# Writing out TensorE's six-turn loop in a three-stage fused kernel

## The chip, the cores and the metric

The kernel runs on one core of a Trainium2 chip. The metric is the device time of one execution in microseconds; lower is better. Five engines of the core work side by side, each with its own instruction stream: TensorE (PE; its weight loads are PEld), VectorE (DVE), ScalarE (ACT), GpSimd (POOL) and SyncE (SP). They meet only through semaphores.

## The reference

```
x = attn(x, weight)                     # 7-tap causal mix over the sequence, softmaxed taps, per head
h1 = x @ moe_w_in                       # 192 -> 2048
g1 = h1 if h1 >= 1, 0 if h1 <= -1, else (h1 + 1)**2 / 4
y  = g1 @ moe_w_out                     # 2048 -> 192
h2 = y @ moe2_w_in                      # 192 -> 2048
g2 = s * relu(h2)**2 + b
out = g2 @ moe2_w_out                   # 2048 -> 192
```

There are 2 sequences of 4096 tokens with 192 channels, all in float32.

## The kernel before

The tokens are cut into 8 blocks of 512 per sequence (`NB = 8`, `T = 512`), both sequences side by side. Channels lie on the partitions. A *phase* is one layer (0 or 1) over one block. It runs over 16 chunks of 128 hidden units. For precision each float32 operand is split into a high part and a low part, and each product is made of several matmuls with 64-row operands. Two of them, on the two halves of the array, run at the same time: below, such a couple is called a *pair*.

In a phase TensorE walks the chunks two at a time. Here this is called a *group*: `up_pair` makes the hidden values of chunks j and j+1 (`up_own` twice, 5 pairs each, L670; `up_other` twice, 4 pairs each, L683) into the two PSUM tensors `h`, and `down` twice (10 pairs each, L717 and L732) multiplies chunks j-2 and j-1 by the second weight matrix into `acc` and `acc_rem`. So a group is 38 pairs, a phase is 8 groups, and the last two chunks of a phase are finished in the first group of the next one. Between the two, ACT makes `r` from `h` (L289 for layer 0, L291 for layer 1), DVE makes `g` (L445, L453; L447 for layer 1), ACT rounds it to `g_hi` (L303, L305) and DVE makes the rest `g_lo` (L463, L466). DVE also does the 7-tap mix of a later block (L498, L502), ACT and DVE split layer 0's result into layer 1's operands, and both drain the accumulators in the first group of a phase (L312 to L316 and L475, L478).

The order is written by hand. Phase (0, block 0) and phase (0, block 1) come first as straight code. Then a loop runs `LOOPS = NB - 2 = 6` times; each turn is one phase of layer 1 and one of layer 0 for a later block. The last two phases, both of layer 1, are straight code again. PE, DVE and ACT each have this loop, as a hardware loop (`Fori`) over a register; SP has one of five turns for its loads and stores. The loops of the engines are not tied to each other by anything but the semaphores of the data. All semaphore counts rise through the whole kernel, and a wait in a loop compares with a value worked out from the loop's register, where one in straight code compares with a constant.

Of the kernel before, what the change touches and what calls it, by code (L numbers as in the profile page):

```python
# [32 lines left out]
def build(nc, x, weight, w1_in, w1_out, w2_in, w2_out, s, b, out):  # L33
# [10 lines left out]
    LOOPS = NB - 2  # L44
# [3 lines left out]
    with ctx:  # L48
# [607 lines left out]
        def _(pe):  # L656
# [85 lines left out]
            def phase(layer, before, S0, P0, xs, split, weights=None):  # L742

                for j in range(0, CH, 2):
                    if weights and j in weights:
                        pe.wait_ge(w1_lo_done, weights[j])
                    up_pair(layer, j, S0 + j, xs, split if j == 0 else None)
                    for d in (j - LAG, j - LAG + 1):
                        if d >= 0:
                            down(layer, d, S0 + d, P0)  # L750
                        elif before is not None:
                            down(before, CH + d, S0 + d, P0 - 1)

            def mixed_split(blk):

                return {"hi": [(x_hi_done[0], blk + 1)], "lo": [(x_lo_done[0], blk + 1)],
                        "rem": [(x_rem_lo_done[0], 2 * (blk + 1))]}

            def y_split(blk):

                return {"hi": [(x_hi_done[1], blk + 1)], "lo": [(x_lo_done[1], blk + 1)],
                        "rem": [(x_rem_lo_done[1], 2 * (blk + 1))]}
# [23 lines left out]
            phase(0, None, 0, 0, X1, first_split, weights)  # L786
            phase(0, 0, CH, 1, X1, mixed_split(1))
            pe.wait_ge(w2_lo_done, N_PARTS)
            with pe.Fori(0, LOOPS) as c:
                S0, P0 = (c + 1) * (2 * CH), (c + 1) * 2  # L790
                phase(1, 0, S0, P0, X2, y_split(c))
                phase(0, 1, S0 + CH, P0 + 1, X1, mixed_split(c + 2))
# [31 lines left out]
```

## Time and profile before

| | us |
|---|---|
| median of 3 runs | 1169.5 (1169.03 to 1171.97) |
| the profiled execution's own time | 1166.02 |
| its span, from the first to the last instruction | 1164.3 |
| mean granted TensorE clock, as a share of full | 0.992 |
| busy: PE / PEld / DVE / ACT | 1126.6 / 983.3 / 947.4 / 630.3 |

The profiled execution took 1.7 us more than its span and 3.5 us less than the median of the runs. Busy time of PE counts the pipelined, modelled length of matmuls, so it shows where PE has work and not how well it is used. Idle time is listed by what ended it; "issue" is idle time for whose end the profile shows no other engine's event.

### The profile page before, as it was taken

Reading aid. Unit: us, or ns where it says so; the run is one execution under the profiler, and the core shown is the slowest. Engines: PE = TensorE matmul, PEld = TensorE weight load, DVE = VectorE, ACT = ScalarE, POOL = GpSimd, SP = SyncE. Lnnn points to the kernel's source line nnn. Section 1 sums busy time; section 2 is a strip of 40 time slices with the busy share of each in tenths; the row PEclk is TensorE's granted clock in tenths of the full one; section 3 lists DMA queues with packets and bytes.
Section 4 is the critical chain, followed back from the end, with each engine's and each line's share of the span. In section 5 each row is a group of like instructions: output and inputs, shape, how many; then the busy total and the mean of one; then the engine's idle time right before and its main releaser. Section 6 shows DMA issues by size and latency. Waiting matters only on the chain.

```text
span 1164.3 us, 23819 instructions
## 1 busy us (share of the span) xinstructions
PE 1126.6 (97%) x9746; PEld 983.3 (84%) x9746; DVE 947.4 (81%) x858; ACT 630.3 (54%) x627; POOL 3.4 (0%) x16
## 2 busy tenths in 40 slices
PE   5998999999899999999999999999998999999998
PEld 3777778888799998888878888899997888888886
DVE  7999988879688887878878798787886978876665
ACT  4546656555455554555555555555554555465554
POOL 1000000000000000000000000000000000000000
PEclk8999999999999999999999999999999999999999
DMA  6002200000000000000000000000000000000000
GB/s 181 1 1 81 75 1 1 29 28 1 3 1 28 28 1 2 1 28 29 1 2 1 28 28 1 2 1 28 28 2 2 1 20 9 2 1 1 28 1 28
DMA packets 12434, 21.52 MB, mean 18 GB/s; under 512 B 1072, under 2 KB 5168, under 8 KB 12336
## 3 DMA queue, kind: packets, MB, share of 16 engines
q1 hardware_dynamic: 12256, 19.99, 5.9%
q8 instruction: 89, 1.46, 0.5%
q14 instruction: 9, 0.07, 0.0%
q0 software_dynamic: 64, 0.00, 0.0%
q10 hardware_dynamic: 16, 0.00, 0.0%
HBM read 13.70 MB, written 6.29 MB: 17 GB/s over the span
## 4 chain that ended last, share of the span: by engine, by line
PE 87%; DVE 8%; issue 4%; ACT 0%; DMA 0%; SPq 0%; DVEq 0%; ACTq 0%
PE acc L717 27%; PE h L670 23%; PE h L683 18%; PE acc_rem L732 18%; DVE g L445 3%; DVE g L453 1%; DVE mixed L502 1%; ACT g_hi L303 0%; DMA xraw_rem<-in_x 0%; DVE mixed_rem L516 0%; DVE mixed L516 0%; DVE up_lo L551 0%; DVE up_rem_lo L551 0%; DVE g_lo L463 0%; DVE dn_lo L551 0%
## 5 line engine op out<-in xcount | busy, mean ns | idle before, releaser
L303 ACT ACTIVATE g_hi<-g 128x1024 fp32r<-128x1024 f32 x128 | 135.8, 1061 | 218.9 <-DVE g L453 218.9
L447 DVE SCALAR_TENSOR_TENSOR g<-r,scale,h 128x1024 f32<-128x1024 f32 x128 | 161.9, 1277 | 89.0 <-ACT r L291 89.0
L305 ACT ACTIVATE g_hi<-g,shift 128x1024 fp32r<-128x1024 f32 x128 | 147.6, 1153 | 116.1 <-PE acc_rem L732 100.9
L717 PE MATMUL acc<-g_hi,dn_hi 64*128 64x512 f32 x1024 | 210.0, 387 | 0.4 <-issue 0.4
L732 PE MATMUL acc_rem<-g_hi,dn_rem 64*128 64x512 f32 x1024 | 209.8, 386 | 0.0
L717 PE MATMUL acc<-g_lo,dn_hi 64*128 64x512 f32 x1024 | 209.8, 386 | 0.0
L732 PE MATMUL acc_rem<-g_lo,dn_rem 64*128 64x512 f32 x1024 | 209.7, 386 | 0.0
L717 PE MATMUL acc<-g_hi,dn_lo 64*128 64x512 f32 x1024 | 209.6, 386 | 0.0
L466 DVE SCALAR_TENSOR_TENSOR g_lo<-g,shift,g_hi 128x1024 fp32r<-128x1024 f32 x128 | 164.1, 1282 | 43.1 <-ACT g_hi L305 42.8
L291 ACT ACTIVATE r<-h 128x1024 f32<-128x1024 f32 x128 | 127.6, 1026 | 129.6 <-PE h L683 117.2
L463 DVE TENSOR_TENSOR g_lo<-g,g_hi 128x1024 fp32r<-128x1024 f32 x128 | 156.7, 1224 | 42.6 <-ACT g_hi L303 42.2
L445 DVE TENSOR_TENSOR g<-h,r 128x1024 f32<-128x1024 f32 x128 | 156.2, 1220 | 21.9 <-ACT r L289 21.6
L289 ACT ACTIVATE r<-h,half 128x1024 f32<-128x1024 f32 x128 | 139.9, 1113 | 37.0 <-PE h L683 31.3
L453 DVE SCALAR_TENSOR_TENSOR g<-r,g 128x1024 f32<-128x1024 f32 x128 | 156.4, 1222 | 2.2
L670 PE MATMUL h<-x_hi,up_hi 64*128 64x512 f32 x512 | 108.0, 399 | 23.8 <-issue 14.0
L717 PEld LDWEIGHTS acc<-g_hi,dn_hi 64*128 64x128 f32 x1024 | 102.0, 184 | 18.4 <-issue 0.8
L717 PEld LDWEIGHTS acc<-g_lo,dn_hi 64*128 64x128 f32 x1024 | 106.2, 184 | 13.1
L732 PEld LDWEIGHTS acc_rem<-g_lo,dn_rem 64*128 64x128 f32 x1024 | 106.2, 184 | 13.1
L732 PEld LDWEIGHTS acc_rem<-g_hi,dn_rem 64*128 64x128 f32 x1024 | 106.1, 184 | 13.0
L717 PEld LDWEIGHTS acc<-g_hi,dn_lo 64*128 64x128 f32 x1024 | 106.2, 184 | 11.8
L670 PE MATMUL h<-x_rem,up_rem_hi 64*128 64x512 f32 x512 | 106.8, 394 | 2.7 <-DVE x_rem L529 2.7
L670 PE MATMUL h<-x_lo,up_hi 64*128 64x512 f32 x512 | 106.8, 394 | 0.4 <-DVE x_lo L521 0.4
(96 smaller groups left out, 1407.2 us busy)
## 6 DMA issues: line engine op xcount, KB each, us to landing
xraw<-in_x SPq DMA_DIRECT2D x7, 518.0 KB, 4.3
out<-res SPq DMA_DIRECT2D x7, 512.0 KB, 3.2
stage<-in_moe_w_out SPq DMA_DIRECT2D x6, 384.0 KB, 3.4
xraw_rem<-in_x SPq DMA_DIRECT2D x14, 129.5 KB, 4.0
out<-res_rem SPq DMA_DIRECT2D x7, 256.0 KB, 3.5
stage<-in_moe_w_in SPq DMA_DIRECT2D x2, 512.0 KB, 5.6
stage<-in_moe_w_in SPq DMA_DIRECT2D x4, 256.0 KB, 5.3
xraw<-in_x SPq DMA_DIRECT2D x1, 512.0 KB, 4.3
```

Of the source, the lines that this page charges most:

```text
L289: nc.scalar.activation(r[k][:], h[k][:], ACT.Relu, scale=0.5, bias=half[:, 0:1]).then_inc(r_ready, 1)
L303: nc.scalar.activation(g_hi[k][:], g[k][:], ACT.Copy).then_inc(hi_ready, 1)
L305: nc.scalar.activation(g_hi[k][:], g[k][:], ACT.Identity, bias=shift[:, 0:1]).then_inc(hi_ready, 1)
L445: nc.vector.tensor_tensor(g[k][:], h[k][:], r[k][:], ALU.max).then_inc(h_used, 1)
L447: nc.vector.scalar_tensor_tensor(g[k][:], r[k][:], scale[:, 0:1], h[k][:], ALU.mult, ALU.mult).then_inc(h_used, 1)
L453: nc.vector.scalar_tensor_tensor(g[k][:], r[k][:], 1.0, g[k][:], ALU.min, ALU.mult).then_inc(g_ready, 1)
L463: nc.vector.tensor_tensor(g_lo[k][:], g[k][:], g_hi[k][:].bitcast(F32), ALU.subtract).then_inc(lo_ready, 1)
L466: nc.vector.scalar_tensor_tensor(g_lo[k][:], g[k][:], shift[:, 0:1], g_hi[k][:].bitcast(F32), ALU.add, ALU.subtract).then_inc(lo_ready, 1)
L670: last = nc.tensor.matmul(h[j % 2][:, t, :], w[rows, cols], v[rows, t, :], start=(n == 0), stop=False)
L683: last = nc.tensor.matmul(h[j % 2][:, t, :], w[rows, cols], v[rows, t, :], start=False, stop=(n == 3))
L717: last = nc.tensor.matmul(acc[:, t, :], w[rows], v[rows, t, :], start=(j == 0 and side == 0 and n == 0), stop=(j == CH - 1 and side == 1 a ...
L732: last = nc.tensor.matmul(acc_rem[:, t, :], both[rows], v[rows, t, :], start=(j == 0 and side == 0 and n == 0), stop=(j == CH - 1 and side ...
```

## The change

TensorE's hardware loop over the six middle turns becomes a loop of the program that builds the kernel: the same instructions are written out six times, with constants in the waits. DVE, ACT and SP keep their loops. No matmul is added, dropped or moved.

```diff
--- before.py
+++ after.py
@@ -786,7 +786,7 @@
             phase(0, None, 0, 0, X1, first_split, weights)
             phase(0, 0, CH, 1, X1, mixed_split(1))
             pe.wait_ge(w2_lo_done, N_PARTS)
-            with pe.Fori(0, LOOPS) as c:
+            for c in range(LOOPS):
                 S0, P0 = (c + 1) * (2 * CH), (c + 1) * 2
                 phase(1, 0, S0, P0, X2, y_split(c))
                 phase(0, 1, S0 + CH, P0 + 1, X1, mixed_split(c + 2))
```

## Rows read from the trace of the kernel before

**Rows 1.** The page: busy time, and the chain that ended last.

```profile
PE 1126.6 (97%) x9746; PEld 983.3 (84%) x9746; DVE 947.4 (81%) x858; ACT 630.3 (54%) x627; POOL 3.4 (0%) x16
...
PE 87%; DVE 8%; issue 4%; ACT 0%; DMA 0%; SPq 0%; DVEq 0%; ACTq 0%
```

**Rows 2.** Waits of PE, in total: us, times, longest us.

```profile
PE h L670 <- issue: 14.0, 5, 3.1
PE h L670 <- DVE g L445: 7.5, 11, 1.8
```

**Rows 3.** The chain in order of time: start us, us, what.

```profile
297.95 2.27 PE h L670 x20
306.56 2.95 issue
...
320.02 2.27 PE h L670 x20
...
440.61 2.27 PE h L670 x20
...
462.38 2.27 PE h L670 x20
...
582.97 2.27 PE h L670 x20
591.58 2.58 issue
...
603.08 2.27 PE h L670 x20
...
723.66 2.27 PE h L670 x20
...
743.98 2.27 PE h L670 x20
...
864.57 2.27 PE h L670 x20
...
886.75 2.27 PE h L670 x20
...
1024.58 2.27 PE h L670 x20
...
1145.45 2.27 PE h L670 x20
```

**Rows 4.** Stretches: busy us (instructions) of each engine, granted clock, DMA share, GB/s.

```profile
309.90:313.30 3.40, 3.40 (x20) 3.13 (x18) 0.92 (x1) 0.00 (x0) 0.00 (x0) 0.51 0.02 5
453.30:456.70 3.40, 3.40 (x18) 3.09 (x17) 0.17 (x1) 0.00 (x0) 0.00 (x0) 0.50 0.00 0
594.20:597.60 3.40, 3.40 (x30) 3.15 (x32) 1.23 (x1) 0.29 (x1) 0.00 (x0) 1.00 0.02 5
876.90:880.30 3.40, 3.40 (x20) 3.02 (x19) 0.54 (x1) 0.00 (x0) 0.00 (x0) 0.55 0.00 0
```

**Rows 5.** Timeline of DVE and ACT around 594 us, with idle before.

```profile
587.34 1.22 DVE L445 TENSOR_TENSOR g<-h,r 128x1024 f32<-128x1024 f32 x1 [0.29 <-ACT r L289]
589.74 1.22 DVE L445 TENSOR_TENSOR g<-h,r 128x1024 f32<-128x1024 f32 x1
592.09 1.22 DVE L453 SCALAR_TENSOR_TENSOR g<-r,g 128x1024 f32<-128x1024 f32 x1
593.44 1.06 ACT L303 ACTIVATE g_hi<-g 128x1024 fp32r<-128x1024 f32 x1 [2.52 <-DVE g L453]
594.62 1.23 DVE L463 TENSOR_TENSOR g_lo<-g,g_hi 128x1024 fp32r<-128x1024 f32 x1 [1.31 <-ACT g_hi L303]
597.75 1.94 ACT L291 ACTIVATE r<-h 128x1024 f32<-128x1024 f32 x2 [3.26 <-PE h L683]
598.91 1.28 DVE L447 SCALAR_TENSOR_TENSOR g<-r,scale,h 128x1024 f32<-128x1024 f32 x1 [3.07 <-ACT r L291]
601.29 1.28 DVE L447 SCALAR_TENSOR_TENSOR g<-r,scale,h 128x1024 f32<-128x1024 f32 x1
```

**Rows 6.** DMA queue of instructions, in 603:731 and in 1016:1150: packets, MB, share.

```profile
q8 instruction: 9, 0.15, 0.5%
...
q8 instruction: 10, 0.16, 0.5%
```

**Rows 7.** Stretches as in rows 4: one inside a turn, one of straight code.

```profile
603.00:731.00 128.00, 128.00 (x1134) 113.20 (x1132) 108.41 (x96) 71.91 (x70) 0.00 (x0) 1.00 0.04 14
1016.00:1150.00 134.00, 134.00 (x1182) 114.91 (x1180) 83.78 (x70) 72.48 (x70) 0.00 (x0) 1.00 0.02 7
```

## The prediction

> **What bounds the kernel now.** I read the page first: PE has work in 97% of the span and the chain that ended last is 87% PE, with 4% that is called issue [rows 1]. DVE is busy 81% and appears in the chain only at the start, where the weights are still being split. So time is gained only where PE stands still, or where its matmuls come more slowly than they could. The list of PE's waits gives the first of these [rows 2]: 14.0 us of issue in five pieces, all before L670, which is the first line of a group. The DVE waits of 7.5 us lie in the two straight phases at the start and in the first group of the loop, which has no jump before it.
>
> The chain in order of time then says where the five pieces are [rows 3]. They begin near 306.6, 449.2, 591.6, 732.3 and 873.2 us, 141 to 143 us apart. A turn of the loop is 16 groups, so this is the step from one turn to the next: six turns have five such steps. Halfway through each turn there is a phase boundary with the same code, the same split waits and the same accumulator waits, and no idle time stands there. The loop's jump back is the one thing that the five places have and the halfway places have not.
>
> Between the steps the groups come at an even pace. Inside a turn, 14 groups lie between 603.08 and 723.66 us: 120.58 / 14 = 8.613 us each. In the straight code at the end, 14 groups lie between 1024.58 and 1145.45: 120.87 / 14 = 8.634 us each [rows 3]. PE is without idle time in both stretches [rows 7], so both are the pace of PE itself, by its two forms of code.
>
> **What a jump back costs.** I take the two groups around each step, from one clean group start to another, and subtract two groups at 8.613 (17.23 us) [rows 3]:
>
> - 297.95 to 320.02: 22.07, over by 4.84
> - 440.61 to 462.38: 21.77, over by 4.54
> - 582.97 to 603.08: 20.11, over by 2.88
> - 723.66 to 743.98: 20.32, over by 3.09
> - 864.57 to 886.75: 22.18, over by 4.95
>
> The sum is 20.3 us. Of this 14.0 is the idle time itself. The steps come in two kinds, near 3.0 and near 4.8, and the granted clock tells them apart. After the first, second and fifth stop the granted clock is 0.51, 0.50 and 0.55 for 3.4 us, which is the lower level of 1.2 GHz; after the third it stays at 1.00 [rows 4], and the fourth step's size puts it with the third. Before each fall PE had stood still for 2.6 to 3.1 us. 3.4 us at half speed lose 1.7 us, so three falls are about 5.0 of the 20.3, and the remaining 1.3 is the first group's slow start. All three parts go with the stop.
>
> **The change part by part.**
>
> *The five jumps go.* -20.3 us. The sixth turn leaves the loop without a jump, and its last group runs at the usual pace, so nothing more is to be had there.
>
> *The register arithmetic and the waits against registers go, and constants come.* These run in PE's instruction stream beside matmuls that are already queued. Their effect is what the two paces show: the straight form is the slower by 8.634 - 8.613 = 0.021 us a group. 6 turns of 16 groups are 96 groups: +2.0 us. The bounds are 0, if the straight layer-0 and layer-1 phases here should run as the loop does, and 2.0 us more, if the form costs layer 0 three times as much; nothing in the rows asks for either. I take 2.0, since the last two phases are written by the same functions and the first of them is the very phase (1, 0) that each turn begins with.
>
> *The instructions must be brought in once more for each turn.* They are already: a stretch of 128 us inside a turn has 9 packets of instructions and one of 134 us in straight code has 10, one in 14.2 and one in 13.4 us, and PE is without idle time through both [rows 6, 7]. A loop whose body were kept would show none. So straight code brings in no more per microsecond than the loop. I cost it at nothing; the cover is that the next piece arrives while PE works through the present one, and if that cover were gone, each of some 60 pieces would cost PE a stop (the second rival).
>
> The Trainium skill ("Runtime: NRT & Kernel Launch", Instruction fetch mechanics) says that instructions are fetched ahead in sequence only and that a taken branch to a target no longer held must wait for a fetch. "Advanced Engine Details and Errata" (Control Flow Timing) gives a compare-and-branch about 108 ns, by which five jumps are an estimated 0.5 us instead of 20.3, and the sum would be a change of +1.5 us. By the first rule the trace agrees, with 2.6 to 3.1 us at each jump; by the second figure alone it does not.
>
> *What is late next.* Without the stop PE asks for its inputs earlier, against engines that keep their loops. I take the step at 591.58, where PE resumed at 594.17, and let it go on at 591.58 [rows 3, 5]. It needs the first `h` tensor free at once: DVE's last read of it ended at 588.56, 3.0 us early. It needs the second after 5 pairs, at 591.58 + 5 x 0.227 = 592.7: DVE ended at 590.96, 1.7 us early. It needs `g_lo` of the last chunk for the second `down`, after 28 pairs, at 597.9: DVE's L463 ends at 595.85, 2.1 us early; ACT's `g_hi` ends at 594.50. ACT's `r` started 3.58 us after PE's group start, so it would start at 595.2, and DVE's L447 1.16 us later at 596.3: DVE is free from 595.85, by 0.5 us. This is the tightest place. A delay there would reach PE only through the second `h`: its L447 ends 8.4 us after the group's start (602.57 - 594.17) and is wanted at 8.61 + 1.13 = 9.75, so 1.3 us more are to spare. The jumps of ACT and DVE are seen here too: ACT's first operation after its own (L303, 593.44) starts 0.1 us after its input is ready at 593.31, and DVE's (L463, 594.62) 0.1 us after `g_hi`. They are hidden behind data waits on which PE's stop has no bearing. So nothing takes the place of the stop, at a price of 0.
>
> **The sum.** -20.3 + 2.0 = -18.3 us. Against the profiled execution, 1166.0 - 18.3 = 1147.7. The median of the runs is 3.5 us above it; if that difference stays, the median becomes 1169.5 - 18.3 = 1151.2. It need not stay whole: which stops are followed by a fall of the clock may differ between executions, and with all five followed by one the saving grows by 2 x 1.7 = 3.4, to 1147.8; with none of them it shrinks by 5.0, to 1156. I say 1151.
>
> **Rivals.**
>
> 1. *The stop moves to another engine.* With PE ahead by 2.6 to 3.1 us at each step, DVE or ACT is late after its own jump. For it: DVE is busy 108.41 of 128 us in a turn, against 83.78 of 134 in the last phases [rows 7], so it has least room just here. Against it: the margins above. It decides from 0.5 + 1.3 = 1.8 us of lateness; if DVE were 3 us late at each step, PE would lose 1.2 five times, 6 us: 1157.
> 2. *Slower: straight code starves.* Six turns of straight code are some 60 pieces of instructions in a row, and if each were late, PE would stop at each. It pays up to a mean stop of 18.3 / 60 = 0.3 us and is a loss beyond; at 0.5 us each the time would be 1181. Against it: 134 us of straight code with 10 pieces show no idle time.
> 3. *The idle time isn't the jump's* but a wait of the program that stays. Then only the form of the code changes, +2.0 us: 1171.5, within 0.3%. Against it: no halfway boundary shows it. The estimate from the page's 108 ns comes out here.
> 4. *The clock falls all the same*, without a stop ahead of it. Three to five falls at 1.7 us bring 5 to 8 us back: 1156 to 1160. Against it: it stayed at 1.00 from 603 to 731 us and through the straight stretch [rows 7].
>
> **How the numbers follow.** The forecast has 0.84, rival 1 has 0.05, rival 2 has 0.03, rival 3 has 0.03 and rival 4 has 0.05. 0.3%, or 3.5 us, is about what a measurement of this kernel can tell from no change. All cases but rivals 2 and 3 are faster beyond it; rival 2 is mostly slower: faster 0.94, same 0.03, slower 0.03. The range runs from 1147, all five clock falls saved and a little of the 2.0 not paid, to 1156, where no fall was there to save or rival 1 or 4 begins.
>
> **What would show it.** In the profile after: no issue waits of PE before L670 between 170 and 1010 us; 96 groups in a row at 8.63 to 8.64 us; a granted clock of 1.00 throughout the middle; about as many instruction packets as before. DVE and ACT keep their shapes but have no idle stretch of 3 to 5 us at the steps. PE waits for DVE (L445, L447, L463) at the steps would speak for rival 1, short idle pieces every 13 us for rival 2, five pieces of 2.6 to 3.1 us left in place for rival 3, a clock of 0.5 without a stop for rival 4. The prediction is wrong if pieces of instructions come late in code that runs straight for 860 us, which no stretch of the kernel before is long enough to show.

## The result and the profile after

| | before | changed |
|---|---|---|
| median of 4 runs, us | 1169.26 (1168.7 to 1171.97) | 1152.1 (1150.71 to 1153.19) |
| ratio | | 0.9848, 95% interval 0.9829 to 0.9867 |
| span of the profiled execution, us | 1164.3 | 1149.0 |
| instructions executed | 23819 | 23218 |

The kernel became 17.2 us faster in the medians, where 18.3 were forecast. The changed kernel's page, busy time and chain, answers to [rows 1]:

```profile
PE 1125.8 (98%) x9746; PEld 951.0 (83%) x9746; DVE 947.9 (83%) x858; ACT 630.8 (55%) x627; POOL 3.4 (0%) x16
...
PE 88%; DVE 8%; issue 3%; ACT 1%; DMA 0%; SPq 0%; DVEq 0%; ACTq 0%
```

The changed kernel's waits of PE (us in total, times, longest) answer to [rows 2]:

```profile
PE h L670 <- DVE g L445: 6.8, 8, 1.8
PE h L769 <- DVE head_taps L597: 3.8, 1, 3.8
```

The 14.0 us of issue before L670 are gone and nothing has taken their place. The waits for DVE that are left lie at the start, and so do the 3% of issue in the chain: between 180 and 1000 us the chain has none. The changed kernel's stretches (columns as in [rows 4]) say the same of the whole middle:

```profile
180.00:1000.00 820.00, 820.00 (x7216) 704.77 (x7214) 693.31 (x613) 456.26 (x440) 0.00 (x0) 1.00 0.04 12
```

820 us without idle time, at full clock. The change can be measured by itself on the 96 middle groups, from the first group of the first turn to the first group behind the last. Timeline of PE, the kernel before:

```profile
167.54 0.39 PE L670 MATMUL h<-x_hi,up_hi 64*128 64x512 f32 x2
...
1015.78 0.40 PE L670 MATMUL h<-x_hi,up_hi 64*128 64x512 f32 x2
```

and the changed kernel:

```profile
169.76 0.39 PE L670 MATMUL h<-x_hi,up_hi 64*128 64x512 f32 x2
...
1000.39 0.40 PE L670 MATMUL h<-x_hi,up_hi 64*128 64x512 f32 x2
```

848.24 us became 830.63: 17.6 less, of 18.3 forecast. But the middle begins 2.2 us later, in code that the diff does not touch. Most of that is one stretch: the group that starts near 94 us starts 0.5 us later than before and the next one 2.8 us. The kernel before and then the changed kernel, 95 to 102 us:

```profile
95.00:102.00 7.00, 5.62 (x47) 4.56 (x48) 5.78 (x7) 3.76 (x5) 0.00 (x0) 1.00 0.88 231
```

```profile
95.00:102.00 7.00, 5.92 (x28) 4.05 (x27) 5.78 (x6) 2.85 (x4) 0.00 (x0) 0.54 0.92 254
```

The granted clock is 0.54 where it was 1.00; both kernels have PE standing still for some 3 us around this point, in pieces, waiting for DVE. So the profile's span fell by 15.3 us and not by 17.6.

### The profile page after: what moved, and what is told of

The parts are those of the page before. It is cut to its first block, busy times and chain, and to the rows that moved or that the text cites. A ratio compares the mean times of both kernels' runs of the same rounds, so it can differ in the third digit from the quotient of the medians.

```text
span 1149.0 us, 23218 instructions
## 1 busy us (share of the span) xinstructions
PE 1125.8 (98%) x9746; PEld 951.0 (83%) x9746; DVE 947.9 (83%) x858; ACT 630.8 (55%) x627; POOL 3.4 (0%) x16
## 4 chain that ended last, share of the span: by engine, by line
PE 88%; DVE 8%; issue 3%; ACT 1%; DMA 0%; SPq 0%; DVEq 0%; ACTq 0%
PE acc L717 28%; PE h L670 23%; PE h L683 18%; PE acc_rem L732 18%; DVE g L445 3%; DVE g L453 1%; DVE mixed L502 1%; DMA xraw_rem<-in_x 0%; ACT g_hi L303 0%; DVE mixed_rem L516 0%; DVE mixed L516 0%; DVE up_lo L551 0%; DVE up_rem_lo L551 0%; DVE g_lo L463 0%; DVE dn_lo L551 0%
## 5 line engine op out<-in xcount | busy, mean ns | idle before, releaser
L447 DVE SCALAR_TENSOR_TENSOR g<-r,scale,h 128x1024 f32<-128x1024 f32 x128 | 161.9, 1278 | 69.5 <-ACT r L291 69.5
L717 PE MATMUL acc<-g_hi,dn_hi 64*128 64x512 f32 x1024 | 204.7, 389 | 0.4 <-issue 0.4
L732 PE MATMUL acc_rem<-g_lo,dn_rem 64*128 64x512 f32 x1024 | 204.6, 388 | 0.0
L732 PE MATMUL acc_rem<-g_hi,dn_rem 64*128 64x512 f32 x1024 | 204.6, 387 | 0.0
L717 PE MATMUL acc<-g_lo,dn_hi 64*128 64x512 f32 x1024 | 204.3, 388 | 0.0
L717 PE MATMUL acc<-g_hi,dn_lo 64*128 64x512 f32 x1024 | 204.0, 387 | 0.0
L717 PEld LDWEIGHTS acc<-g_lo,dn_hi 64*128 64x128 f32 x1024 | 100.1, 185 | 17.0
L732 PEld LDWEIGHTS acc_rem<-g_lo,dn_rem 64*128 64x128 f32 x1024 | 100.5, 185 | 16.5
L732 PEld LDWEIGHTS acc_rem<-g_hi,dn_rem 64*128 64x128 f32 x1024 | 100.0, 184 | 16.6
L670 PE MATMUL h<-x_hi,up_hi 64*128 64x512 f32 x512 | 103.7, 395 | 9.2 <-DVE g L445 6.8
L717 PEld LDWEIGHTS acc<-g_hi,dn_lo 64*128 64x128 f32 x1024 | 100.3, 185 | 11.7
L670 PE MATMUL h<-x_rem,up_rem_hi 64*128 64x512 f32 x512 | 103.0, 392 | 2.4 <-DVE x_rem L529 2.4
L670 PE MATMUL h<-x_lo,up_hi 64*128 64x512 f32 x512 | 102.9, 392 | 0.6 <-DVE x_lo L521 0.4
```

The lines of the kernel that those rows point to most:

```text
L447: nc.vector.scalar_tensor_tensor(g[k][:], r[k][:], scale[:, 0:1], h[k][:], ALU.mult, ALU.mult).then_inc(h_used, 1)
L670: last = nc.tensor.matmul(h[j % 2][:, t, :], w[rows, cols], v[rows, t, :], start=(n == 0), stop=False)
L717: last = nc.tensor.matmul(acc[:, t, :], w[rows], v[rows, t, :], start=(j == 0 and side == 0 and n == 0), stop=(j == CH - 1 and side == 1 a ...
L732: last = nc.tensor.matmul(acc_rem[:, t, :], both[rows], v[rows, t, :], start=(j == 0 and side == 0 and n == 0), stop=(j == CH - 1 and side ...
```

## The experiments

Theory: a jump back costs PE a fetch, since the start of its long body is no longer at hand; and straight code is a little slower in every group because its waits take another form. Rivals: any jump costs it, or any turn; the slower pace belongs to running straight; the cost is handed on to DVE or ACT. "Middle" is the stretch of 96 groups measured above.

**The turns in loops that run once.** The changed kernel with:

```diff
-            for c in range(LOOPS):
+            for turn in range(LOOPS):
+                with pe.Fori(turn, turn + 1) as c:
...
```

> Each of the six turns stands in a loop of its own that runs once, so PE jumps back nowhere, but the waits compare with registers again, as in the kernel before. If the slower pace of straight code (8.634 us a group against 8.613) comes from the form of the waits with constants, the 96 middle groups take 96 x 8.613 + about 1 = 828 us from the first group of the first turn to the first group after the last, against 830.6 in the changed kernel and 848.2 before, and the time is 2 us below the changed kernel, near 1150. If the slower pace comes from running straight (instructions brought in, addresses), it stays at 8.634 and the time at 1152. If a loop costs something even without a jump back, idle time of PE shows at six places.

Measured: 1154.1 us (1150.21 to 1155.84), ratio 0.9877 (0.986 to 0.9895), no issue wait of PE before L670. The experiment missed its aim: the page counts 23236 instructions, 18 more than the changed kernel, where the kernel before has 601 more; with bounds that are known, the waits had got constants after all and were those of straight code. The time differs from the changed kernel's no more than that kernel's own runs do. What it shows is that a loop's entry and exit without a jump back cost nothing: its middle took 829.9 us, as in the second profile of the changed kernel below. The pace, in its chain in order of time, is that of straight code, (1129.63 - 179.97) / 110 groups = 8.633 us:

```profile
179.97 2.27 PE h L670 x20
...
1129.63 2.27 PE h L670 x20
```

**Two turns in a body.** The kernel before with its loop of three runs over two turns:

```diff
-            with pe.Fori(0, LOOPS) as c:
+            with pe.Fori(0, LOOPS // 2) as double:
+                for odd in range(2):
+                    c = double * 2 + odd
...
```

> The loop runs three times over a body of two turns: two jumps back instead of five, each over twice as many instructions. If a jump costs a fetch of its target whatever the body's length, two stops of 2.6 to 3.1 us are left, and with what hangs on them (3.0 us, or 4.8 where the clock falls) the time is 5 to 10 above the kernel with registers and no jump: 1155 to 1160, at a pace of 8.613 us a group. If the stop grew with the length of the body, two stops of 5 to 6 us would be left, and the time would be about 1163. If the stops were not the jump's but belonged to each turn, there would be five.

Measured: 1157.98 us (1157.09 to 1159.62), ratio 0.991 (0.9894 to 0.9927). Its chain in order of time:

```profile
436.04 2.27 PE h L670 x20
...
444.66 2.68 issue
...
457.59 2.27 PE h L670 x20
...
715.99 2.27 PE h L670 x20
...
724.61 2.93 issue
...
739.28 2.27 PE h L670 x20
```

Two jumps, two stops of 2.7 and 2.9 us, the size they had over a body half as long. So the cost goes by the jump, not by the turn nor by the body's length. With the clock behind them they cost 21.55 - 17.23 = 4.3 and 23.29 - 17.23 = 6.1.

The traces also hold the jump itself: the record of the branch at the end of the loop, L789, on PE's sequencer (PEldq), which reads the instruction stream. In the kernel before (how many, then ns at least, median, at most), and then the queue of instructions while the third branch lasts, 590.6 to 593.9 us:

```profile
L789 PEldq COMPARE_BRANCH  x6: 79/3390/3759, 305.6 to 1015.0; - x6
```

```profile
q8 instruction: 1, 0.02, 1.8%
```

The five branches that are taken last 3.3 to 3.8 us and the sixth, which leaves the loop, 0.08. The four profiles of kernels in which PE jumps back over turns (the kernel before twice, this one, and the last kernel of "The order of the waits") have 17 such jumps. In every one a packet of instructions starts 0.9 to 1.1 us after the branch began, and the branch ends 1.4 to 1.5 us after that packet has come: where the packet takes longer, so does the branch. So the jump does wait for a fetch. The third one began at 590.61 and PE's matmuls went on to 591.58: about 1 us of them was queued, and only the rest shows as idle time.

**Short jumps.** The changed kernel with, behind each turn:

```diff
+                with pe.Fori(0, 4):
+                    pe.wait_ge(w2_lo_done, N_PARTS)
```

> The changed kernel with a tiny loop behind each written-out turn: one wait that has long been met, run four times, so three short jumps back at each of six places, eighteen in all. If the cost is that the target is no longer at hand, these jumps cost nothing that shows: 1152, no idle time of PE. If any jump back costs 2.6 us or more, 18 of them cost 47 us or more: about 1199. If the cost is a flush of what is queued, about 1 us at each of the six places shows: 1158.

Measured: 1160.51 us (1159.22 to 1161.03), ratio 0.9929 (0.9912 to 0.9945). Waits of PE: 

```profile
PE h L670 <- issue: 2.8, 6, 0.5
```

I had forecast nothing, and 0.5 us of idle time shows at each place for three jumps and four waits: far from 18 stops of 2.6, but near what I had given to a flush (1158). That nearness is in part chance: the middle is 8.0 us longer than the changed kernel's (838.6 against 830.6), and the six groups with the little loops account for half of it, while the other groups take 8.68 us here instead of 8.64, away from any jump. Four rounds of that little loop are also simply work for PE's sequencer, 1.4 us of it (308.6 to 310.0 us) against about 1 us of queued matmuls. So it was made smaller: the kernel of the next experiment, with a loop of two, which is one short jump at each place.

> The kernel with the chain wait first, and one short jump back behind each written-out turn (a loop of two over one wait that has long been met): six jumps, like for like with the five of the kernel before but for the distance. If only the distance is dear, PE has no idle time of issue there and each of the six groups stays within 0.1 us of 8.613: 1147 to 1148. If a jump in itself is dear, six stops of about 2.6 us: 1163 or more.

Measured: 1149.34 us in one run, span 1147.6, no issue wait before L670. That is above the 1147 to 1148 forecast, and 0.8 us above the profiled execution of the same kernel without these jumps (1148.55). The middle is 828.4 us, against 827.9 without the six jumps; one of the six groups took 8.77, more than the 0.1 us allowed. Chain around the first jump, and the branches of the little loops, six taken and six not:

```profile
301.46 2.27 PE h L670 x20
310.08 2.34 PE h L670 x20
318.76 2.27 PE h L670 x20
```

```profile
L793 PEldq COMPARE_BRANCH  x12: 76/142/233, 309.2 to 999.0; - x12
```

17.30 us for two groups, where 17.23 is the undisturbed value and the far jumps made it 20.1 to 22.2 [rows 3]. A near jump that is taken lasts 0.21 to 0.23 us, where a far one lasts 3.3 to 3.8. One jump like for like, but near: 0.4 us in all six together. What is dear is the distance.

**The order of the waits.** The changed kernel, in `down`:

```diff
+                if not first:
+                    pe.wait_ge(main_step, 2 * S)
                 pe.wait_ge(hi_ready, S + 1)
                 pe.wait_ge(lo_ready, S + 1)
...
                     if side == 1:
                         pe.wait_ge(main_step, 2 * S + 1)
-                    elif not first:
-                        pe.wait_ge(main_step, 2 * S)
```

> The changed kernel with the order of the waits at the head of down turned round: the wait for the matmuls before (main_step) is put first and those for hi_ready and lo_ready behind it. In the changed kernel a separate wait instruction holds main_step and lo_ready and the next weight load only hi_ready, and once in each group the weight loads behind it come late and 6 pairs lose 3 to 10 ns each. If that is the 0.021 us a group, and the order decides which wait rides on the weight load, the pace goes to 8.613 in all 128 groups: 2.4 us less, near 1149.5. If the order changes nothing in the form, or the pace has another cause, it stays at 8.634 and at 1152.

Measured: 1148.04 us (1147.53 to 1148.67), ratio 0.9819 (0.9803 to 0.9836). The weight loads around the start of the second `down` of a group, in the changed kernel (start us, us):

```profile
358.07 0.20 PEld L732 LDWEIGHTS acc_rem<-g_hi,dn_rem 64*128 64x128 f32 x2
358.30 0.20 PEld L732 LDWEIGHTS acc_rem<-g_lo,dn_rem 64*128 64x128 f32 x2
358.58 0.21 PEld L717 LDWEIGHTS acc<-g_hi,dn_hi 64*128 64x128 f32 x2
358.75 0.19 PEld L717 LDWEIGHTS acc<-g_hi,dn_lo 64*128 64x128 f32 x2
```

and with the chain wait first (second profile of that kernel):

```profile
358.06 0.19 PEld L717 LDWEIGHTS acc<-g_lo,dn_hi 64*128 64x128 f32 x2
358.29 0.19 PEld L732 LDWEIGHTS acc_rem<-g_hi,dn_rem 64*128 64x128 f32 x2
358.52 0.19 PEld L732 LDWEIGHTS acc_rem<-g_lo,dn_rem 64*128 64x128 f32 x2
358.75 0.19 PEld L717 LDWEIGHTS acc<-g_hi,dn_hi 64*128 64x128 f32 x2
```

In the first, the load that begins a new chunk comes 0.28 us after the one before it instead of 0.23. The trace has a separate wait instruction there, at 358.51 us, that holds `main_step` (the matmuls just ahead) and `lo_ready`; it passes only when those have ended, and the load behind it is late by 0.05 us. The next load has caught up, but a few pairs behind it lose 3 to 10 ns each, some 20 ns in all, which is the difference between the two paces. With the wait for `main_step`, the chain wait, written first it rides on the load itself, and the separate instruction, at 358.06, holds `hi_ready` and `lo_ready`, which are true by then. No load is late any more, and all groups take 8.613 us: the chain of the second profile of it gives (998.78 - 180.52) / 95 = 8.613. In the loop of the kernel before, with registers, the trace has `main_step` on the load too, and its groups took 8.613 as well.

```profile
180.52 2.27 PE h L670 x20
...
998.78 2.27 PE h L670 x20
```

Is it the number of waits or which one stands alone? The changed kernel with only this:

```diff
-                pe.wait_ge(hi_ready, S + 1)
                 pe.wait_ge(lo_ready, S + 1)
```

> The changed kernel with its old order of waits, but without the wait for hi_ready, which lo_ready implies: two waits at the head of down where there were three. If what costs is that the separate wait instruction holds main_step, which comes true only when the pair before has ended, the order of lo_ready before main_step keeps it there, and the pace stays at 8.633 us or more, the time near 1152. If what costs is the number of waits, the pace goes to 8.613 and the time to 1148 as with the chain wait first.

Measured: 1152.92 us (1151.86 to 1153.55), ratio 0.9861 (0.9845 to 0.9878); the late load is still there (358.53, then 358.82):

```profile
358.53 0.20 PEld L731 LDWEIGHTS acc_rem<-g_lo,dn_rem 64*128 64x128 f32 x2
358.82 0.21 PEld L716 LDWEIGHTS acc<-g_hi,dn_hi 64*128 64x128 f32 x2
```

The separate instruction holds `main_step` alone here. So the number of waits is not it. Last, the new order in the kernel before, loop kept:

> The kernel before, with its loop, and only the order of the waits at the head of down turned round. If the order matters only where waits compare with constants, the groups outside the loop go from 8.634 (8.68 in the second profile) to 8.613 and those inside stay: 0.5 to 1.5 us less than before, 1168, and the five stops stay with their 14 us, so that the order is worth nothing near what the jumps are. It is also one more look at the start: in three profiles of kernels that loop, the first turn begins at 167.6 to 167.8 us with no fall of the clock near 96 us, in ten of kernels that are written out it begins at 169.4 to 170.9 with one. If this goes with the loop, it is 167.6 to 167.8 here as well; if it goes by chance or with the order of waits, it may be 169.4 or more.

Measured: 1169.37 us (1165.47 to 1170.81), ratio 1.0004 (0.999 to 1.0018): no difference, below the 0.5 to 1.5 us forecast. All groups, in and out of the loop, are at 8.613 here, but five stops of 14.3 us in total remain, and in its profile the clock fell after three of them, once for twice as long.

**VectorE's jump.** The kernel with the chain wait first, and in DVE's part:

```diff
-            with dve.Fori(0, LOOPS) as c:
-                S0, P0 = (c + 1) * (2 * CH), (c + 1) * 2
+            with dve.Fori(0, LOOPS // 3) as triple:
+                for c in (triple * 3, triple * 3 + 1, triple * 3 + 2):
+                    S0, P0 = (c + 1) * (2 * CH), (c + 1) * 2
...
```

> The kernel with the chain wait first, and VectorE's loop with three turns in its body: it jumps back once, over some 670 instructions, where the loop before jumps five times over some 224. If a jump is dear only when its body is too long to be kept, as on PE with some 2500, and VectorE keeps fewer, VectorE now stands still for 2.6 to 3.5 us at its one jump, near 585 us, and PE, with 1.8 us to spare, waits 1 to 2 us there once: 1149 to 1150. If only PE's jumps are dear, nothing shows: 1148.

Measured: 1147.31 us in one run, span 1145.6, middle 828.0 us: PE lost nothing. Neither theory as written was quite right: VectorE's jump was dear, and yet nothing showed. Queues of the kernel before, 310 to 1010 us (packets, MB, share):

```profile
q1 hardware_dynamic: 3808, 7.12, 3.4%
q8 instruction: 58, 0.95, 0.6%
```

and with DVE's longer body, 310 to 990 us, and then 583.5 to 590 us, around its jump:

```profile
q1 hardware_dynamic: 3808, 7.12, 3.5%
q8 instruction: 48, 0.79, 0.5%
q14 instruction: 10, 0.08, 0.0%
```

```profile
q14 instruction: 2, 0.02, 1.0%
q8 instruction: 1, 0.02, 0.9%
```

In the kernel before no packet comes on q14 for 700 us: the bodies of DVE and ACT, 224 and 199 instructions, are brought in once and kept (with both written out, q14 carries the packets of both). With three turns in DVE's body, 662 instructions, they come again all the time, and two at the jump. DVE's sequencer does stand still there: its branch is at 583.6 us and the first instruction of the next turn at 586.6, 2.9 us after the branch ended, where it is 0.3 us in the kernel before, whose body is a third as long:

```profile
L630 DVEq FUSED_REGOPS  x2: 74/74/74, 171.6 to 586.6; - x2
L630 DVEq COMPARE_BRANCH  x2: 55/64/74, 583.6 to 997.0; - x2
```

So a far jump is no peculiarity of PE, and on DVE the cost begins somewhere between 224 and 662 instructions. But DVE's timeline shows no stop of its work:

```profile
584.59 1.22 DVE L453 SCALAR_TENSOR_TENSOR g<-r,g 128x1024 f32<-128x1024 f32 x1
587.12 1.23 DVE L463 TENSOR_TENSOR g_lo<-g,g_hi 128x1024 fp32r<-128x1024 f32 x1 [1.31 <-ACT g_hi L303]
```

Its next input, ACT's `g_hi`, is ready at 587.00. DVE had 2.2 us of queued work at the jump (583.6 to 585.8) and then 1.3 us of waiting for data, and the fetch fits in there with 0.4 us to spare. PE has about 1 us queued and no wait for data at its jump, so it shows.

**All engines written out**, on the same kernel (`for c in range(LOOPS)` on DVE and ACT too).

> The kernel with the chain wait first, and VectorE's and ScalarE's loops over the six turns written out too. If their jumps are hidden behind data waits, as the rows of before say, this gives nothing: 1148, with the same 8.613 us a group. If they cost PE something at the five steps, it is up to 1 us faster. If three engines that bring in straight code get in each other's way, idle time of PE shows and it is slower than 1150.

Measured: 1148.06 us (1147.78 to 1150.84), ratio 0.9825 (0.9805 to 0.9846). Nothing to be had, and nothing lost: the jumps of DVE and ACT were hidden.

**Second profiles.** The kernel before:

> The kernel before once more, for a second profile. Five stops of 2.6 to 3.1 us at the same places and 8.613 us a group between them are expected. What is asked is which stops are followed by a fall of the clock: if that belongs to the place, the first, second and fifth again; if it changes between executions, others, and with four or five of them the span comes 2 to 3.4 us above the 1164.3 of the first profile, which would account for the 3.5 us by which the runs lay above it. A fall near 96 us, which the profile of the changed kernel has and that of the kernel before has not, may or may not appear: if it does, it has nothing to do with the change.

Measured: 1166.74 us, span 1165.0. Stretches behind the five jumps:

```profile
310.20:313.50 3.30, 3.30 (x18) 3.24 (x16) 0.67 (x1) 0.00 (x0) 0.00 (x0) 0.50 0.00 0
451.90:455.30 3.40, 3.40 (x30) 3.24 (x32) 1.23 (x1) 0.15 (x1) 0.00 (x0) 1.00 0.02 5
593.50:596.80 3.30, 3.30 (x20) 3.19 (x18) 0.75 (x1) 0.00 (x0) 0.00 (x0) 0.50 0.00 0
736.90:740.20 3.30, 3.30 (x19) 3.08 (x18) 0.00 (x0) 0.00 (x0) 0.00 (x0) 0.50 0.00 0
877.90:881.30 3.40, 3.40 (x30) 3.22 (x32) 1.23 (x1) 0.22 (x1) 0.00 (x0) 1.00 0.02 5
```

Again three falls, but behind the first, third and fourth, where it was the first, second and fifth [rows 4]. So which stop is followed by a fall belongs to the execution, not to the place. Its groups outside the loop took (1146.13 - 1024.61) / 14 = 8.680 us, where they had taken 8.634 in the first profile:

```profile
1024.61 2.27 PE h L670 x20
...
1146.13 2.27 PE h L670 x20
```

The late load does not cost the same in each execution. The changed kernel:

> The changed kernel again, for its time beside the next kernel on one chip and a second profile. 1151 to 1153. The fall of the clock near 96 us may be there or not; its groups of 8.66 to 8.69 us among those of 8.633 should stand at other places, if they come from how the waits happen to fall.

Measured: 1152.81 us (1150.04 to 1155.76), ratio 0.9864 (0.9839 to 0.989). In the profile the middle took 829.9 us with all groups at 8.633; the first profile's had 830.6, with some of 8.66 to 8.67. The fall near 96 us was there again. Beside it, the kernel with the chain wait first:

> The kernel with the chain wait first again, beside the changed kernel. 1148, that is 0.3% to 0.4% below the changed kernel, of which 2.7 us are the 128 groups at 8.613 instead of 8.634 and the rest is groups that come later still in the changed kernel; and less spread between the runs.

Measured: 1148.06 us (1147.52 to 1148.59), ratio 0.9823 (0.981 to 0.9837); middle 827.9 us. Its runs lie within 1.1 us of each other, those of the changed kernel within 5.7. The medians are 4.8 us apart, the spans of the two profiles only 1.7 (1148.5 and 1146.8): the rest of the 4.8 lies in two executions of the changed kernel, 1155.3 and 1155.8 us, that have no trace. One of them has the same mean clock, 0.994, as the profiled one of 1150.3, so it isn't the clock. 96 groups at 8.680 instead of 8.633 would be an estimated 4.5 us; that they ran so is not shown.

## Why the prediction held

*What bounds the kernel, and that the five stops are the jump's:* right. The stops vanished with the jumps, fell from five to two with their number (2.7 and 2.9 us), and did not appear for a near jump. That the cost is the fetch of a target no longer held is seen in the trace: a packet of instructions inside each of the 17 far branches, and DVE's jump, 0.3 us over 224 instructions and 2.9 over 662. PE's own delay was not varied between near (a few instructions) and far (2570), so the distance at which it begins there stays open. The Trainium skill's rule ("Runtime: NRT & Kernel Launch", Instruction fetch mechanics) agrees. The 108 ns that the Trainium skill gives in "Advanced Engine Details and Errata" (Control Flow Timing) fit none of PE's branches here: not taken they last 67 to 88 ns, taken and near 208 to 233, far 3273 to 3759.

*-20.3 us for the jumps:* right. The middle without jumps and without the slower form is that of the kernel with the chain wait first, 827.9 us, and 848.2 - 827.9 = 20.3.

*The slower form, +2.0 us:* right in sign, a little small in size. The prediction laid it on the form of the code as a whole; the experiments narrow it to where the wait for `main_step` stands. With the chain wait first the middle is 827.9, so the form cost 830.6 - 827.9 = 2.7 us in one execution and 829.9 - 827.9 = 1.9 in the other. I had bounded it by 0 and 4.0, and took it for a fixed rate: it isn't one. The same form ran at 8.680 in the second profile of before, which over 96 groups would be 6.4 us.

*Nothing in its place at DVE and ACT:* right. The tightest place was given 0.5 us of room; the changed kernel's DVE timeline shows 0.20 of idle time there, before L447:

```profile
588.84 1.23 DVE L463 TENSOR_TENSOR g_lo<-g,g_hi 128x1024 fp32r<-128x1024 f32 x1 [1.31 <-ACT g_hi L303]
590.27 1.28 DVE L447 SCALAR_TENSOR_TENSOR g<-r,scale,h 128x1024 f32<-128x1024 f32 x1 [0.20 <-ACT r L291]
```

So L447 still waits for ACT's `r`, as forecast, and not for DVE's work before it, but with 0.3 us less to spare. Writing out DVE and ACT gave nothing either.

*The instructions at no cost:* right: 49 packets in the 700 us from 310 to 1010, against 58 before, nine fewer with the four jumps in that time gone. Nothing starved.

*The clock (part of the 20.3):* right that a fall comes behind a stop and goes with it, and that its number varies. What I left out is that the stops at the start, which stay, can be followed by one as well: near 96 us it cost the changed kernel most of the 2.2 us by which its middle starts later. The sum had no term for it. That is a term of chance, not of the change, as far as this shows (below).

*From the profile to the median:* here the forecast was partly lucky. For the profiled execution it said 1147.7 us, and 1150.7 was measured, 3.0 more: 2.2 from the later start of the middle, which the prediction held at nothing, and 0.7 from the slower form. For the median it said 1151.2, and 1152.1 was measured, only 0.9 more, because the 3.5 us by which the median lay above the profiled execution shrank to 1.4 in the changed kernel. Why it shrank is not shown. The number of falls of the clock may account for some of it. Of 33 runs of before beside the experiments (without one of 1275 us at a clock of 0.845), the 17 with a mean granted clock of 0.991 or 0.992 took 1166.6 to 1169.8 us and the 9 with 0.986 to 0.988 took 1169.8 to 1171.7; 0.003 x 1168 is 3.5 us of work lost by the mean clock. This is argued, since those runs have no timeline.

## What to carry to other kernels

Look at what stands between the turns of a hardware loop on the engine that bounds the kernel: if the record of its branch lasts microseconds (here 3.3 to 3.8 with a body of 2570 instructions) and the profile shows idle time with no releaser at each turn, write it out, or put more turns into a body; the loops of engines that have work queued or wait for data there can stay. Written-out waits are constants and can be merged differently: look at which wait stands in a separate instruction, and if it is the one for the engine's own last result, try writing that one first, so that it rides on the next weight load. And count a stop of the matmul engine with what the clock may add behind it: here 2.6 to 3.1 us of stop cost 2.9 to 6.1.

## What the runs showed that was not expected

- The mere order of three waits was worth 4.8 us in the medians on one chip (1152.81 to 1148.06), 1.7 of it seen in the two profiles. The eight runs of that kernel lie within 1147.5 to 1148.7 us and the eight of the changed kernel within 1150.0 to 1155.8. The same instructions without it ran at 8.633, 8.66 to 8.67 or 8.68 us a group in different executions; what decides between these is open.
- In all ten profiles of kernels in which PE jumps back over no turn the clock fell near 96 us, for 3.4 or 6.8 us, in none of three profiles of kernels with PE's loop and the old order of waits. The loop with the new order of waits has the fall too (granted clock 0.72 from 93 to 105 us, against 1.00 in the kernel before), so it doesn't go with the loop as such. Why stops of the same length are followed by a fall in one place and not in another was not settled; at the jumps one of 2.65 us was followed by a fall and one of 2.84 was not.
- The first load of weights took 6.2 to 6.4 us in the four profiles of kernels with PE's loop and 6.9 to 9.2 in the other ten. The first group starts at 16.2 to 16.6 us in the former and 16.6 to 17.6 in the latter. A longer program may lie in memory so that the first loads are slower; that wasn't tried.
- With three turns in its body, VectorE fetched instructions all the time and its sequencer stood 2.9 us at the jump, and the kernel lost nothing by it.
